# Moving value, inverse and weight transfers between the steps of a delta-rule scan

## The chip, the cores and the metric

The kernel runs on one core of a Trainium2 chip. The metric is the device time of one execution in microseconds (us).

## The reference

Attention with a delta-rule state over 32 (batch, head) pairs, 768 tokens and head size 48, and then two feed-forward layers over 3072 tokens, 384 features and 2048 hidden units. All is fp32.

```python
for t in range(S):                       # k_n: normalized keys
    y[:, :, t] = einsum('bhd,bhde->bhe', q[:, :, t], state)
    v_old = einsum('bhde,bhd->bhe', state, k_n[:, :, t])
    state = state + beta_t * einsum('bhd,bhe->bhde', k_n[:, :, t], v_t - v_old)
x = y as tokens x features
h = x @ w_in;  g = (a0 + a1*h + a2*h^2 + a3*h^3) / (1 + |b0|*|h| + |b1|*h^2 + 1e-6);  x = g @ w_out
h = x @ w2_in; r = max(h, 0);  result = (r * r) @ w2_out
```

## The kernel before

**The scan.** Tokens are cut into 48 chunks ("groups") of 64 tokens, 12 for each of 4 batches; a group holds 4 head pairs. Four groups are a quad (12 quads, 384 KB of keys, 384 KB of values, 768 KB of turned keys and queries each), eight are a round (6 rounds). Inside a chunk the recurrence becomes a triangular system. Its 32 x 32 diagonal blocks are inverted in place, a round at a time: round 0 on DVE ahead of the loop, rounds 1 to 5 on POOL (`invert`, L393 to L418, with L393 the first operation of a round). The rest is matmul work on PE in a loop of 50 steps, `for n in range(LAST_MM)`, which each engine runs in its own order with semaphores between them. In step n PE starts z of group n (L505), does y and the state of group n-2 (L549, L552), the cross product (L515), m and q of group n-1 (L535), the turned state (L563), the end of z (L521), and the key products of a group some 20 ahead (L484). ACT in the same step takes the products of a former step (L664), z_first (L672), the new state (L686, L687), the cross product (L678), y (L695) and the state (L709); at its end, in some steps, it spreads keys (L643, L645), squares and roots them (L623, L630). The cross product of a step on PE waits for z_first of the same step on ACT. In steps 2 to 7 the keys of half a quad are spread at the end of the step: in step 6 those of quad 7.

**The transfers.** All loads, and the stores of blocks and inverses, are issued from SP, in program order, with their waits in the same order; the stores of y go from ACT. For each step SP runs, in this order: `load_cross` and `load_q` (L308, L292), `load_kq` (L248), `store_n` (L266, L270), `store_inverse(r)` (L287), `load_blocks(r)` (L282), `load_inverse(h)` (L319), `load_k` (L236), `load_v` (L242), weights. `store_inverse(r)` waits for POOL's round r and stands in step `INV_OUT[r]`, that is 6, 13, 20, 27 and 34 for r = 1 to 5. `load_blocks(r)` brings round r to POOL, for r = 2 in step 6 and for r = 5 in step 27, each after the stores (`store_n`) of its quads. `load_kq(7)` stands in step 6, `store_n(11)` in step 26, values of quad 11 in step 34, `load_cross(11)` and `load_inverse(11)` in step 41. The rounds lie in three slots of 1024 columns in `shared[0]`.

**The feed-forward.** A layer is 96 units, 16 blocks of 128 hidden units for each of 6 tiles of 512 tokens. Weights, x and g are split in a high and a low part, and a unit has 9 matmuls up (L1123 to L1125) and 9 down (L1137 to L1139). Raw weights come in a ring of 4 slots of 768 columns in the same `shared[0]`; ACT splits off the high part (L1160), DVE the low one (L1247), into `weights`, which lies where quads 4 to 7, keys and queries were. In the first layer unit n goes through ACT (squares, L1171 to L1177), POOL (denominator, L1341, L1348), ACT (a guess at its reciprocal by Ln and Exp, L1184, L1188), DVE (head, L1270), POOL (L1355), DVE (L1275, L1282), and `up(n)` needs unit n-5 done (`g_lo_ready`). Nine weights (`PRE`) are split in steps 40 to 48 of the scan, the others in the first tile, one each unit. Up-projections of units 0 to 2 lie inside steps 46 to 48.

```python
if n == FF_LOADS:                        # 37
    ff.load_ab(sp)
    ff.load_weights(sp, 0)
    ff.load_x(sp, 0)
    for i in range(1, ff.W_SLOTS):
        ff.load_weights(sp, i)
if 0 <= n - FF_LOADS - 2 < ff.PRE:       # steps 39 to 47
    ff.load_weights(sp, n - FF_LOADS - 2 + ff.W_SLOTS)
```

From the fifth weight on `load_weights` waits on SP until DVE has split the former tenant of the slot.

Of the kernel before, what the change touches and what calls it, by code (L numbers as in the profile page):

```python
# [32 lines left out]
def build_attention(nc, dims, memory, banks, kq_in, k_in, v_in, beta_in, blocks_dram, inverse_dram, cross_dram, ff, x_out):  # L33
# [16 lines left out]
    RING = 32  # L50
# [2 lines left out]
    TWICE = (2, 8)  # L53
    LEAD = UPFRONT + TWICE[1] - TWICE[0]
    LAST_MM = GROUPS + 2
    FF_LOADS, FF_SPLIT, FF_X = GROUPS - 11, GROUPS - 8, (41, 43, 45)
    STORES = 16 * (SUB + 2)
    LOADS = 16 * (SUB + 3)
    INV_OPS = 2 * BL - 2
# [34 lines left out]
    with ExitStack() as ctx:  # L94
# [137 lines left out]
        def _(sp):  # L232
# [6 lines left out]
            def load_v(h):  # L239
                if h >= RING // 4:  # L240
                    sp.wait_ge(ys_done, 4 * h + 4 - RING)
                sp.dma_start(ring(h)[:, :, :, 0:D].rearrange("r g p d -> r (g p) d"),  # L242
                             v_in[:, QP * h:QP * h + QP, :]).then_inc(v_loaded[h % (RING // 4)], 16)
# [101 lines left out]
            load_blocks(1)  # L345
            load_k(6)
            load_k(7)
            load_v(2)
            for n in range(LAST_MM):
                for h in range(2, QUADS):  # L350
                    if n == 4 * h - 3:
                        load_cross(h)
                for h in range(6, QUADS):
                    if n == (2 * h - 8 if h < 9 else 4 * h - 26):
                        load_kq(h)
                for h in range(4, QUADS):
                    if n == step_of_quad(h):
                        store_n(h)
                for r in range(1, ROUNDS):
                    if n == INV_OUT[r]:  # L360
                        store_inverse(r)
                for r in range(2, ROUNDS):
                    if n == step_of_quad(2 * r + 1) + 1:
                        load_blocks(r)
                for h in range(2, QUADS):
                    if n == max(4 * h - 3, INV_OUT[h // 2]):
                        load_inverse(h)
                for h in range(8, QUADS):
                    if n == 4 * h - 26:
                        load_k(h)  # L370
                for h in range(3, QUADS):
                    if n == 4 * h - 10:
                        load_v(h)
                if n == FF_LOADS:
                    ff.load_ab(sp)
                    ff.load_weights(sp, 0)
                    ff.load_x(sp, 0)
                    for i in range(1, ff.W_SLOTS):
                        ff.load_weights(sp, i)
                if 0 <= n - FF_LOADS - 2 < ff.PRE:  # L380
                    ff.load_weights(sp, n - FF_LOADS - 2 + ff.W_SLOTS)
            ff.sync(sp)

        @block.gpsimd
# [233 lines left out]
        def _(act):  # L618
# [116 lines left out]
            for n in range(LAST_MM):  # L735
                if n > 0 and end_group(n - 1) is not None:
                    take_n(end_group(n - 1))
                if n < GROUPS:
                    take_z_first(n)
                if n in FF_X:  # L740
                    ff.split_x_hi(act, FF_X.index(n), 0)
                spread = (n + 1 + LEAD) // 2 if n > TWICE[1] and n % 2 == 1 and end_group(n + 1) is not None else None
                if spread is not None:
                    spread_keys(spread, (0,))
# [22 lines left out]
                        roots(norm_chunk(h))  # L767
                if n == 4 * QUADS - 24:
                    act.preload_act_table_set("natural_log_exp_and_others")
                if 0 <= n - FF_SPLIT < ff.PRE:  # L770
                    ff.split_weights_hi(act, n - FF_SPLIT)
                if n == GROUPS - 1:
                    ff.take_h(act, 0)
                if n == GROUPS:
# [5 lines left out]
        def _(dve):  # L780
# [158 lines left out]
            for n in range(LAST_MM):  # L939
# [20 lines left out]
                for h in range(2, QUADS):  # L960
                    if n == (1 if h == 2 else 4 * h - 5):
                        scale_v(h)
                if n == FF_SPLIT:
                    ff.coef_bounds(dve)
                if 0 <= n - FF_SPLIT < ff.PRE:
                    ff.split_weights_lo(dve, n - FF_SPLIT)
                if n in FF_X:
                    ff.split_x_lo(dve, FF_X.index(n), 0)
            ff.vector(dve, ys_done, GROUPS)


def build_feed_forward(nc, ctx, rows, moe_in, moe_out, coef_dram, memory, banks, x_first, x_second, out):
# [9 lines left out]

    LAG_RECIP, LAG_HEAD, LAG_LOW, LAG_DOWN = 1, 2, 3, 5
    H_BANKS, DEEP, TRIPLE, SHORT = 5, 4, 3, 2
    W_SLOTS, W_AHEAD, PRE = 4, 3, 9
    EARLY = {UNITS - 7: 0, UNITS - 5: 1, UNITS - 3: 2}

    def sem(name):
# [62 lines left out]
        return ps_h[n % H_BANKS]  # L1051

    def load_ab(sp):
        sp.dma_start(ab, coef_dram).then_inc(ab_loaded, 16)

    def load_weights(sp, i):
        m, f, slot = i // FT, i % FT, i % W_SLOTS
        if i >= W_SLOTS:  # L1060
            sp.wait_ge(w_lo_ready, i - W_SLOTS + 1)
        sp.dma_start(w_raw[:, slot, 0:D_MODEL].rearrange("p (k n) -> p k n", k=KT),
                     w_in_dram[m][:, :, f * P:(f + 1) * P]).then_inc(w_loaded[slot], 16)
        sp.dma_start(w_raw[:, slot, D_MODEL:2 * D_MODEL], w_out_dram[m][:, f, :]).then_inc(w_loaded[slot], 16)
# [88 lines left out]

    def split_weights_hi(act, i):
        f = i % FT
        act.wait_ge(w_loaded[i % W_SLOTS], 32 * (i // W_SLOTS) + 32)
        if i >= FT:
            act.wait_ge(h_ready, UNITS - FT + f + 1)
            act.wait_ge(down_done, UNITS - FT + f + 1)
        act.activation(weights[:, f, 0:2 * D_MODEL], w_raw[:, i % W_SLOTS], ACT.Copy).then_inc(w_hi_ready, 1)  # L1160

    def split_x_hi(act, k, tile):
        act.wait_ge(x_loaded, 16 * (tile + 1))
# [80 lines left out]
    def split_weights_lo(dve, i):  # L1244
        f = i % FT
        dve.wait_ge(w_hi_ready, i + 1)
        dve.tensor_tensor(weights[:, f, 2 * D_MODEL:4 * D_MODEL], w_raw[:, i % W_SLOTS],  # L1247
                          weights[:, f, 0:2 * D_MODEL].bitcast(F32), ALU.subtract).then_inc(w_lo_ready, 1)

    def split_x_lo(dve, k, tile):  # L1250
# [203 lines left out]
```

## Time and profile before

| | |
|---|---|
| median of 3 runs | 1114.39 us (1114.38 to 1116.54) |
| the profiled execution | 1114.34 us |
| its span, first to last instruction | 1112.6 us |
| PE busy | 1094.1 us (98%) |
| DVE, ACT, POOL busy | 678.0, 650.8, 509.2 us |
| mean granted TensorE clock | 0.994 |
| key products and scan loop | to about 327 us |
| the twelve feed-forward tiles | from there to the end |

Busy times count an engine from the start of an instruction to its modelled end; matmuls overlap, so their durations add up to more than the time. The granted clock is in parts of 2.4 GHz: 1.00 is the full and 0.50 the lower level.

### The profile page before, as it was taken

To read this page: it belongs to the slowest core of one execution; us is meant where nothing else is said; L and a number is where in the kernel's file an instruction comes from. 1 tells how busy PE (TensorE), PEld (TensorE's weight loads), DVE (VectorE), ACT (ScalarE), POOL (GpSimd) and SP (SyncE) were. 2 spreads that over 40 slices of the span, in tenths; PEclk is the share of its full clock that TensorE was granted. 3 is DMA by queue.
4 is the path that set the end of the run, shared out by engine and by line. 5 is a ranking of instruction groups with operands and counts; after the bars stand their busy time and mean duration, and the time that the engine had idled before them with its cause. 6 is when DMAs were issued, how large, how long until landed. Compare 5 with 4: busy or idle time off the path is not lost.

```text
span 1112.6 us, 18161 instructions
## 1 busy us (share of the span) xinstructions
PE 1094.1 (98%) x6372; PEld 944.5 (85%) x6372; DVE 678.0 (61%) x1088; ACT 650.8 (58%) x1275; POOL 509.2 (46%) x626
## 2 busy tenths in 40 slices
PE   8899999999999999999999999999999999999998
PEld 6699999999987788888888888888888888888887
DVE  6987564434559989787888879854333333434332
ACT  5566666544669777787877778653333323333322
POOL 5087888783039977887777878500000000000000
PEclk9799999999999999999999999999999999999999
DMA  8948887555531110100101002140100101010000
GB/s 193 204 84 182 165 180 151 117 94 149 135 107 57 44 57 1 32 27 1 57 1 57 1 22 93 43 128 1 57 1 9 49 1 57 0 57 1 1 29 29
DMA packets 173658, 74.41 MB, mean 67 GB/s; under 512 B 136000, under 2 KB 161728, under 8 KB 172608
## 3 DMA queue, kind: packets, MB, share of 16 engines
q1 hardware_dynamic: 163968, 68.54, 25.6%
q10 hardware_dynamic: 9600, 4.72, 1.7%
q8 instruction: 51, 0.84, 0.3%
q14 instruction: 39, 0.32, 0.1%
HBM read 52.27 MB, written 20.71 MB: 66 GB/s over the span
## 4 chain that ended last, share of the span: by engine, by line
PE 89%; DVE 6%; issue 2%; DMA 1%; POOL 1%; SPq 1%; ACT 0%; POOLq 0%; DVEq 0%; ACTq 0%
PE ps L1137 11%; PE ps L1139 11%; PE ps L1138 11%; PE ps L1123 11%; PE ps L1125 11%; PE ps L1124 11%; PE ps L505 3%; PE ps L484 3%; PE ps L549 3%; PE ps L535 3%; PE ps L552 3%; PE ps L515 3%; PE ps L521 2%; PE ps L467 1%; PE ps L563 1%
## 5 line engine op out<-in xcount | busy, mean ns | idle before, releaser
L1123 PE MATMUL ps<-x_split,weights 128*128 128x512 f32 x576 | 225.0, 391 | 3.8 <-DVE g_lo L1282 2.9
L1137 PE MATMUL ps<-g_hi,weights 128*128 128x512 f32 x576 | 224.1, 389 | 0.1
L1124 PE MATMUL ps<-x_split,weights 128*128 128x512 f32 x576 | 224.1, 389 | 0.0
L1125 PE MATMUL ps<-x_split,weights 128*128 128x512 f32 x576 | 224.1, 389 | 0.0
L1138 PE MATMUL ps<-g_lo,weights 128*128 128x512 f32 x576 | 224.1, 389 | 0.0
L1139 PE MATMUL ps<-g_hi,weights 128*128 128x512 f32 x576 | 224.1, 389 | 0.0
L1292 DVE TENSOR_TENSOR common<-common 128x512 f32<-128x512 f32 x96 | 66.4, 691 | 135.0 <-ACT common L1196 133.4
L1202 ACT ACTIVATE g_hi<-common 128x512 fp32r<-128x512 f32 x96 | 60.8, 633 | 141.8 <-PE ps L1139 137.3
L1123 PEld LDWEIGHTS ps<-x_split,weights 128*128 128x128 f32 x576 | 108.1, 188 | 27.9 <-DVE g_lo L1282 4.6
L1341 POOL TENSOR_SCALAR common<-common,b_abs 128x512 f32<-128x512 f32 x96 | 75.8, 789 | 116.1 <-ACT common L1171 116.1
L1355 POOL TENSOR_TENSOR common<-common,g_hi 128x512 f32<-128x512 f32 x96 | 124.4, 1296 | 9.5 <-DVE g_hi L1270 9.5
L1348 POOL TENSOR_TENSOR common<-common 128x512 f32<-128x512 f32 x96 | 124.5, 1297 | 8.0
L1137 PEld LDWEIGHTS ps<-g_hi,weights 128*128 128x128 f32 x576 | 108.1, 188 | 22.9 <-issue 0.4
L1125 PEld LDWEIGHTS ps<-x_split,weights 128*128 128x128 f32 x576 | 108.1, 188 | 22.5
L1138 PEld LDWEIGHTS ps<-g_lo,weights 128*128 128x128 f32 x576 | 108.1, 188 | 22.5
L1139 PEld LDWEIGHTS ps<-g_hi,weights 128*128 128x128 f32 x576 | 108.1, 188 | 22.4
L1124 PEld LDWEIGHTS ps<-x_split,weights 128*128 128x128 f32 x576 | 108.1, 188 | 22.2
L1196 ACT ACTIVATE common<-ps 128x512 f32<-128x512 f32 x96 | 57.4, 598 | 103.8 <-PE ps L1125 103.5
L1299 DVE TENSOR_TENSOR g_lo<-common,g_hi 128x512 fp32r<-128x512 f32 x96 | 66.3, 691 | 61.5 <-PE ps L1139 61.5
L1171 ACT ACTIVATE common<-ps 128x512 f32<-128x512 f32 x96 | 57.3, 597 | 72.6 <-PE ps L1125 71.9
L1258 DVE TENSOR_TENSOR common<-common,ps 128x512 f32<-128x512 f32 x96 | 65.8, 685 | 52.5 <-ACT common L1177 51.7
L408 POOL TENSOR_TENSOR shared<-shared,scan_x 128x30 f32<-128x30 f32 (+9 forms) x150 | 84.1, 560 | 11.7
(121 smaller groups left out, 1917.4 us busy)
## 6 DMA issues: line engine op xcount, KB each, us to landing
scan_late<-kq_in SPq DMA_DIRECT2D x10, 768.0 KB, 5.4
scan_late<-kq_in SPq DMA_DIRECT2D x16, 384.0 KB, 4.7
shared<-w_in SPq DMA_DIRECT2D x32, 192.0 KB, 2.5
shared<-w_out SPq DMA_DIRECT2D x32, 192.0 KB, 2.6
x_first<-y_t ACTq DMA_DIRECT2D x24, 192.0 KB, 2.9
shared<-x_first SPq DMA_DIRECT2D x6, 768.0 KB, 5.8
x_second<-shared SPq DMA_DIRECT2D x6, 768.0 KB, 4.2
shared<-x_second SPq DMA_DIRECT2D x6, 768.0 KB, 5.9
```

The source lines that it names most:

```text
L408: step = pool.tensor_tensor(rest, rest, part, ALU.add)
L1123: pe.matmul(bank(n), lo, x_hi[:, slot, k, :], start=(k == 0), stop=False)
L1124: pe.matmul(bank(n), hi, x_lo[:, slot, k, :], start=False, stop=False)
L1125: mm = pe.matmul(bank(n), hi, x_hi[:, slot, k, :], start=False, stop=(k == KT - 1))
L1137: pe.matmul(ps_y[m], lo, g_hi[:, d, :], start=(f == 0), stop=False)
L1138: pe.matmul(ps_y[m], hi, g_lo[:, s, :], start=False, stop=False)
L1139: mm = pe.matmul(ps_y[m], hi, g_hi[:, d, :], start=False, stop=(f == FT - 1))
L1292: dve.tensor_tensor(q[:, n % DEEP, :], r, r, ALU.mult).then_inc(act_ready, 1)
L1299: dve.tensor_tensor(g_lo[:, n % TRIPLE, :], q[:, d, :], g_hi[:, d, :].bitcast(F32), ALU.subtract).then_inc(g_lo_ready, 1)
L1341: pool.tensor_scalar(den_part[:, s, :], h_sq[:, s, :], b_abs[:, 1:2], ONE_EPS, ALU.mult, ALU.add).then_inc(den_part_ready, 1)
L1348: pool.tensor_tensor(q[:, n % DEEP, :], den_part[:, s, :], b0_h[:, s, :], ALU.add).then_inc(q_ready, 1)
L1355: pool.tensor_tensor(prod[:, n % SHORT, :], q[:, n % DEEP, :], g_hi[:, n % DEEP, :].bitcast(F32), ALU.mult).then_inc(prod_ready, 1)
```

## The change

SP asks for the values of quads 3 to 7 directly behind those of quad 2, ahead of its loop, where they stood in steps 2, 6, 10, 14 and 18. `store_inverse(r)` is the first thing in its step. The small coefficients and weight 0 are asked for in step 31, weight 1 in 32, x in 33, weights 2 and 3 in 35 and 36, 4 and 5 in 37, 6 and 7 in 39, and 8 to 13 in 42 to 47. Weights 0 to 9 are split in steps 33, 34, 36, 37 and 41 to 46, the three parts of x in steps 38, 39 and 40. Weights 2 and 3 come into the slots of 0 and 1, so that the other two slots, where round 5 of the inverses lies, are first written by weights 4 and 5; `raw_slot`, `raw_former` and `raw_loads` say which slot, whose split frees it, and how many loads it has had. `PRE` is 10: one weight less is split in the first tile.

```diff
@@ -53,7 +53,11 @@
     TWICE = (2, 8)
     LEAD = UPFRONT + TWICE[1] - TWICE[0]
     LAST_MM = GROUPS + 2
-    FF_LOADS, FF_SPLIT, FF_X = GROUPS - 11, GROUPS - 8, (41, 43, 45)
+
+    W_LOADS = {31: (0,), 32: (1,), 35: (2,), 36: (3,), 37: (4, 5), 39: (6, 7), 42: (8,), 43: (9,), 44: (10,), 45: (11,),
+               46: (12,), 47: (13,)}
+    W_SPLITS = {33: 0, 34: 1, 36: 2, 37: 3, 41: 4, 42: 5, 43: 6, 44: 7, 45: 8, 46: 9}
+    X_LOAD, X_SPLITS = 33, (38, 39, 40)
     STORES = 16 * (SUB + 2)
     LOADS = 16 * (SUB + 3)
     INV_OPS = 2 * BL - 2
@@ -345,8 +349,12 @@
             load_blocks(1)
             load_k(6)
             load_k(7)
-            load_v(2)
+            for h in range(2, RING // 4):
+                load_v(h)
             for n in range(LAST_MM):
+                for r in range(1, ROUNDS):
+                    if n == INV_OUT[r]:
+                        store_inverse(r)
                 for h in range(2, QUADS):
                     if n == 4 * h - 3:
                         load_cross(h)
@@ -356,9 +364,6 @@
                 for h in range(4, QUADS):
                     if n == step_of_quad(h):
                         store_n(h)
-                for r in range(1, ROUNDS):
-                    if n == INV_OUT[r]:
-                        store_inverse(r)
                 for r in range(2, ROUNDS):
                     if n == step_of_quad(2 * r + 1) + 1:
                         load_blocks(r)
@@ -368,17 +373,15 @@
                 for h in range(8, QUADS):
                     if n == 4 * h - 26:
                         load_k(h)
-                for h in range(3, QUADS):
+                for h in range(RING // 4, QUADS):
                     if n == 4 * h - 10:
                         load_v(h)
-                if n == FF_LOADS:
+                if n == min(W_LOADS):
                     ff.load_ab(sp)
-                    ff.load_weights(sp, 0)
+                for i in W_LOADS.get(n, ()):
+                    ff.load_weights(sp, i)
+                if n == X_LOAD:
                     ff.load_x(sp, 0)
-                    for i in range(1, ff.W_SLOTS):
-                        ff.load_weights(sp, i)
-                if 0 <= n - FF_LOADS - 2 < ff.PRE:
-                    ff.load_weights(sp, n - FF_LOADS - 2 + ff.W_SLOTS)
             ff.sync(sp)
 
         @block.gpsimd
@@ -737,8 +740,8 @@
                     take_n(end_group(n - 1))
                 if n < GROUPS:
                     take_z_first(n)
-                if n in FF_X:
-                    ff.split_x_hi(act, FF_X.index(n), 0)
+                if n in X_SPLITS:
+                    ff.split_x_hi(act, X_SPLITS.index(n), 0)
                 spread = (n + 1 + LEAD) // 2 if n > TWICE[1] and n % 2 == 1 and end_group(n + 1) is not None else None
                 if spread is not None:
                     spread_keys(spread, (0,))
@@ -767,8 +770,8 @@
                         roots(norm_chunk(h))
                 if n == 4 * QUADS - 24:
                     act.preload_act_table_set("natural_log_exp_and_others")
-                if 0 <= n - FF_SPLIT < ff.PRE:
-                    ff.split_weights_hi(act, n - FF_SPLIT)
+                if n in W_SPLITS:
+                    ff.split_weights_hi(act, W_SPLITS[n])
                 if n == GROUPS - 1:
                     ff.take_h(act, 0)
                 if n == GROUPS:
@@ -960,12 +963,12 @@
                 for h in range(2, QUADS):
                     if n == (1 if h == 2 else 4 * h - 5):
                         scale_v(h)
-                if n == FF_SPLIT:
+                if n == min(W_SPLITS):
                     ff.coef_bounds(dve)
-                if 0 <= n - FF_SPLIT < ff.PRE:
-                    ff.split_weights_lo(dve, n - FF_SPLIT)
-                if n in FF_X:
-                    ff.split_x_lo(dve, FF_X.index(n), 0)
+                if n in W_SPLITS:
+                    ff.split_weights_lo(dve, W_SPLITS[n])
+                if n in X_SPLITS:
+                    ff.split_x_lo(dve, X_SPLITS.index(n), 0)
             ff.vector(dve, ys_done, GROUPS)
 
@@ -982,7 +985,7 @@
 
     LAG_RECIP, LAG_HEAD, LAG_LOW, LAG_DOWN = 1, 2, 3, 5
     H_BANKS, DEEP, TRIPLE, SHORT = 5, 4, 3, 2
-    W_SLOTS, W_AHEAD, PRE = 4, 3, 9
+    W_SLOTS, W_AHEAD, PRE = 4, 3, 10
     EARLY = {UNITS - 7: 0, UNITS - 5: 1, UNITS - 3: 2}
 
     def sem(name):
@@ -1051,14 +1054,26 @@
         return ps_h[n % H_BANKS]
 
+    def raw_slot(i):
+        return i if i < 2 else (i + 2) % W_SLOTS
+
+    def raw_former(i):
+
+        return {2: 0, 3: 1}.get(i, i - W_SLOTS if i >= 6 else None)
+
+    def raw_loads(i):
+
+        return 1 if i < 2 else (i + 2) // W_SLOTS + (raw_slot(i) < 2)
+
+
 
     def load_ab(sp):
         sp.dma_start(ab, coef_dram).then_inc(ab_loaded, 16)
 
     def load_weights(sp, i):
-        m, f, slot = i // FT, i % FT, i % W_SLOTS
-        if i >= W_SLOTS:
-            sp.wait_ge(w_lo_ready, i - W_SLOTS + 1)
+        m, f, slot = i // FT, i % FT, raw_slot(i)
+        if raw_former(i) is not None:
+            sp.wait_ge(w_lo_ready, raw_former(i) + 1)
         sp.dma_start(w_raw[:, slot, 0:D_MODEL].rearrange("p (k n) -> p k n", k=KT),
                      w_in_dram[m][:, :, f * P:(f + 1) * P]).then_inc(w_loaded[slot], 16)
         sp.dma_start(w_raw[:, slot, D_MODEL:2 * D_MODEL], w_out_dram[m][:, f, :]).then_inc(w_loaded[slot], 16)
@@ -1153,11 +1168,11 @@
 
     def split_weights_hi(act, i):
         f = i % FT
-        act.wait_ge(w_loaded[i % W_SLOTS], 32 * (i // W_SLOTS) + 32)
+        act.wait_ge(w_loaded[raw_slot(i)], 32 * raw_loads(i))
         if i >= FT:
             act.wait_ge(h_ready, UNITS - FT + f + 1)
             act.wait_ge(down_done, UNITS - FT + f + 1)
-        act.activation(weights[:, f, 0:2 * D_MODEL], w_raw[:, i % W_SLOTS], ACT.Copy).then_inc(w_hi_ready, 1)
+        act.activation(weights[:, f, 0:2 * D_MODEL], w_raw[:, raw_slot(i)], ACT.Copy).then_inc(w_hi_ready, 1)
 
     def split_x_hi(act, k, tile):
         act.wait_ge(x_loaded, 16 * (tile + 1))
@@ -1244,7 +1259,7 @@
     def split_weights_lo(dve, i):
         f = i % FT
         dve.wait_ge(w_hi_ready, i + 1)
-        dve.tensor_tensor(weights[:, f, 2 * D_MODEL:4 * D_MODEL], w_raw[:, i % W_SLOTS],
+        dve.tensor_tensor(weights[:, f, 2 * D_MODEL:4 * D_MODEL], w_raw[:, raw_slot(i)],
                           weights[:, f, 0:2 * D_MODEL].bitcast(F32), ALU.subtract).then_inc(w_lo_ready, 1)
 
     def split_x_lo(dve, k, tile):
```

## Rows read from the trace of the kernel before

**Rows 1.** Busy time by stretch: us, PE, PEld, DVE, ACT, POOL, clock, DMA share, GB/s
```profile
60.00:70.00 10.00, 8.67 (x86) 8.54 (x86) 8.00 (x19) 5.46 (x14) 8.75 (x16) 1.00 0.01 3
...
110.00:120.00 10.00, 10.00 (x102) 9.77 (x101) 6.59 (x15) 6.91 (x21) 8.82 (x16) 1.00 1.14 211
```

**Rows 2.** SP queue, loop steps 4 to 6: start, us, engine, line, operation
```profile
74.10 0.34 SPq L248 DMA_DIRECT2D scan_late<-kq_in  x1
...
91.57 0.48 SPq L248 DMA_DIRECT2D scan_late<-kq_in  x1
...
95.00 0.34 SPq L287 DMA_DIRECT2D inverse_blocks<-shared  x1
95.52 0.34 SPq L282 DMA_DIRECT2D shared<-blocks  x1
```

**Rows 3.** Busy time of a stretch full of loads, columns as in group 1
```profile
97.00:99.00 2.00, 2.00 (x22) 2.00 (x22) 0.94 (x5) 2.00 (x8) 0.00 (x0) 1.00 0.86 295
```

**Rows 4.** ACT timeline, end of step 6; in brackets idle before, and releaser
```profile
96.80 0.72 ACT L643 ACTIVATE scan_late<-scan_late,scan_common 96x512 f32<-96x512 f32 x1 [0.97 <-DMA scan_late<-kq_in]
```

**Rows 5.** PE timeline, step 7
```profile
99.47 0.92 PE L515 MATMUL ps<-scan_common,scan_late 128*96 128x96 f32 x8
```

**Rows 6.** POOL timeline, the first operation of four rounds
```profile
53.88 2.36 POOL L393 TENSOR_TENSOR shared<-shared,scan_common 128x1024 f32<-128x1024 f32 x1 [34.89 <-DMA shared<-blocks]
...
100.28 2.36 POOL L393 TENSOR_TENSOR shared<-shared,scan_common 128x1024 f32<-128x1024 f32 x1 [5.31 <-DMA shared<-blocks]
...
139.84 2.35 POOL L393 TENSOR_TENSOR shared<-shared,scan_common 128x1024 f32<-128x1024 f32 x1
...
222.75 2.36 POOL L393 TENSOR_TENSOR shared<-shared,scan_common 128x1024 f32<-128x1024 f32 x1 [5.75 <-DMA shared<-blocks]
```

**Rows 7.** SP queue, loop step 34
```profile
261.61 0.34 SPq L287 DMA_DIRECT2D inverse_blocks<-shared  x1
262.00 0.43 SPq L242 DMA_DIRECT2D scan_x<-v_in  x1
```

**Rows 8.** ACT timeline, last operation of step 36 and the first weight split
```profile
261.46 0.49 ACT L709 ACTIVATE scan_common<-ps 96x384 f32<-96x384 f32 x1 [0.35 <-PE ps L563]
...
280.43 0.83 ACT L1160 ACTIVATE weights<-shared 128x768 fp32r<-128x768 f32 x1
```

**Rows 9.** PE timeline, cross product of step 37, starts of steps 42 to 44
```profile
264.38 0.84 PE L515 MATMUL ps<-scan_common,scan_late 128*96 128x96 f32 x8
...
285.43 1.06 PE L505 MATMUL ps<-scan_common 128*128 128x96 f32 x8
...
290.33 1.06 PE L505 MATMUL ps<-scan_common 128*128 128x96 f32 x8
...
296.15 1.13 PE L505 MATMUL ps<-scan_x,scan_common 128*128 128x96 f32 x8 [0.76 <-DMA scan_common<-inverse_blocks]
```

**Rows 10.** DVE, ACT and PE timelines, start of the feed-forward
```profile
324.24 0.96 DVE L1247 TENSOR_TENSOR weights<-shared,weights 128x768 fp32r<-128x768 f32 x1 [0.97 <-ACT weights L1160]
...
330.93 0.64 ACT L1184 ACTIVATE common<-common 128x512 f32<-128x512 f32 x1 [0.98 <-POOL common L1348]
...
338.29 0.50 PE L1123 MATMUL ps<-x_split,weights 128*128 128x512 f32 x1 [2.39 <-DVE g_lo L1282]
```

**Rows 11.** PE timeline, first matmul of two up-projections in the first tile
```profile
354.74 0.39 PE L1123 MATMUL ps<-x_split,weights 128*128 128x512 f32 x1
...
368.24 0.50 PE L1123 MATMUL ps<-x_split,weights 128*128 128x512 f32 x1 [0.25 <-DVE g_lo L1282]
```

**Rows 12.** PE timeline and stretches with the granted clock, before and after gaps
```profile
15.65 7.31 PE L484 MATMUL ps<-scan_late 96*128 96x128 f32 x64
...
25.87 5.47 PE L484 MATMUL ps<-scan_late 96*128 96x128 f32 x32 [2.91 <-ACT scan_late L645]
...
28.00:29.00 1.00, 1.00 (x7) 1.00 (x6) 0.89 (x4) 0.00 (x0) 0.00 (x0) 0.50 1.39 112
...
338.00:340.00 2.00, 1.71 (x7) 1.43 (x8) 1.98 (x4) 2.00 (x5) 2.00 (x3) 1.00 0.04 8
```

## The prediction

> **What bounds the kernel now.** I read the page first, then PE busy by stretches, then the PE, ACT, POOL and SP timelines of the places where PE is not full. In the scan a 10 us stretch has PE busy for all 10.00 [rows 1], and from step 9 to the first up-projection I find one PE stall only, at step 44. So an edit inside the scan gives time back only at a PE gap, and it costs time as soon as PE has to wait. The gaps that the change can touch are: 0.76 us at step 44, ended by the DMA that brings inverses [rows 9]; 2.39 us before unit 6 of the feed-forward, ended by a DVE g_lo [rows 10]; and the units around 360 us, whose starts are more than a PE-bound unit apart [rows 11]. SP is one queue in program order: a wait at its head holds back everything behind it. That is where the new order must be followed.
>
> **Early values.** Quads 4 to 7 leave their places in steps 6, 10, 14 and 18 and go behind quad 3, which SP already issued before the first wait of the loop. DMA is idle from 60 to 70 us (share 0.01) and SP's next load, of keys and queries of quad 6, goes out at 74.10 [rows 1, 2]. One such transfer has 384 KB; at the 295 GB/s that a load stretch moves [rows 3] four need 5.3 us, at half that rate 10.7 us: done by about 66 to 71 us. Cost nothing; without that gap it would be up to 10 us on quad 6. They gain nothing either: no PE gap stands where they stood.
>
> **Stores first.** INV_OUT is unchanged, so only the order inside a step changes. It matters at step 6. Before, SP issued keys and queries of quad 7 at 91.57, then waited for POOL, stored round 1 at 95.00 and loaded the blocks of round 2 at 95.52 [rows 2]. Now the store's wait is ahead of that load: it goes out at about 95.39, 3.8 us later, and the blocks at about 96.0, 0.5 us later. ACT has no room for this: it already sat 0.97 us until that load landed, at 96.80 [rows 4], after a flight of 5.2 us, and PE's next L515 started late behind it [rows 5]. Store, quad 7 and blocks are 512, 768 and 512 KB, 1.31 MB up to the end of quad 7 and 1.83 MB in all. At 295 GB/s [rows 3] that is 4.4 and 6.2 us of data. Of quad 7's old flight of 5.2 us 2.7 were data at that rate, so at most 2.5 lie around it; I take 1.8. Then quad 7 lands near 95.0 + 1.8 + 4.4 = 101.2 (4.4 late) and the blocks near 103.0 (POOL took up round 2 at 100.28 [rows 6], so 2.8 late). Bounds: quad 7 3.8 (same flight) to 5.1; blocks 0.5 (only the issue) to 5.2 (a whole flight behind quad 7). ACT is in order: behind the spread of keys stand the roots of quad 7 and the copies of step 7, so PE stops before L515 of step 7 for about 4.2 us. From there PE is 4.2 late. POOL runs its rounds back to back, so it stays 2.8 late; its one later wait, for the blocks of round 5 (restart at 222.75 [rows 6]), is behind a store of quad 11 that now is 4.2 late, about 3.0 in all. At step 13 the cross blocks and queries of quad 4 wait for the store too, three steps ahead of their use: nothing.
>
> **Weights from step 31 on.** Weights 0 and 1 and x are asked for in slots whose rounds were stored long ago. Weight 2 is asked for at step 35, behind the store of round 5 at step 34. SP came past that store only at 261.61 [rows 7], when POOL was done. ACT began its take_state of step 36 at 261.46 [rows 8], ended it near 261.9 and would turn to the split of weight 2 there. With POOL 3.0 late the store goes out at 264.6; then the values of quad 11, then both halves of weight 2 (the values were issued 0.39 us behind the store [rows 7]). The three make 1.31 MB, again 4.4 + 1.8: weight 2 lands 6.2 us after the end of the inversion (bounds: 4.0, an issue at 1.4 and the 2.6 of a transfer that overlaps all others; 8.0, the same data at the 211 GB/s of a mixed stretch [rows 1]), so at 270.8. Then split 0.74 (from its start to the next op's) and z_first 0.49 on ACT: PE's L515 of step 37 can start at about 272.1. It started at 264.38 [rows 9]: 7.7 late, of which 4.2 are the old delay and 3.5 a second stall. Queued behind the wait on ACT are z_first, the state and the y of step 37; PE waits for them. The other splits lie as those of steps 40 to 46 did, at 0.83 us on an ACT with idle time in each step [rows 8]: nothing, as long as their weights are there, and 3, 4 to 9 are asked for a step or more ahead.
>
> **What comes back.** The inverses of quad 11 were behind two weight waits; at step 41 none is there now. Steps 42 and 43 take 4.90 and 5.82 us [rows 9]: 0.9 back. Steps 47 and 48 lose their splits on ACT (0.74 each) and DVE. DVE's last split ran at 324.24, ahead of all its work for unit 0; from it the chain goes over head 0, POOL's product 0 and q 1 to ACT's Ln of unit 1 at 330.93 (0.98 idle for POOL), and, links later, to PE at 338.29 [rows 10]. With the splits gone head 0 is bounded by ACT's guess, 2.0 earlier; ACT is bounded by y of the last chunk and gains 1.35; prod 1 and so unit 6 about 1.4 (bounds 0.7, one split, and 2.4, the whole gap). Ten instead of nine weights split early takes one DVE split (0.96 [rows 10]) and one ACT split out of the first tile. Three units ran 368.24 - 354.74 = 13.50 [rows 11]; the four before ran 354.74 - 338.29 = 16.45, 4.11 each, so 3 x 4.11 = 12.33: 1.2 lost to DVE. I take all of it as back, since DVE also starts the tile 1.4 earlier; bound below 0.9.
>
> **Sum.** +7.7 - 0.9 - 1.4 - 1.2 = +4.2 on the span of 1112.6: 1116.8. The profiled execution took 1114.34, 1.74 more than its span, and lies 0.05 from the median of the runs, so 1118.5.
>
> **Clock.** The granted clock fell to 0.50, the lower of its two levels, at 28 to 29 us, after PE had been idle 2.91 us, and 32 matmuls took 5.47 us; after the 2.39 us gap at 338 it stayed at 1.00 [rows 12]. My two gaps (4.2 and 3.5) are longer than both. At the full level the 64 matmuls before took 7.31 [rows 12], so 32 take 3.6 and a fall costs 1.9. I count none in the sum: these gaps lie in dense work, as the one at 338 did, and not in the thin start. The Trainium skill, "TensorE: Matmul & The Clock Gate", section "Why this matters for your kernels", asks that PE not idle between bursts of matmuls because the clock then goes back to 1.2 GHz. By it each of the two gaps would cost a stretch at the lower level; the trace agrees at 28 us and not at 338.
>
> **The rivals.**
> 1. The clock falls after one or both gaps. For it: both are longer than the one that was followed by a fall, and the first is in matmuls of the same shape. A fall at step 7 is not absorbed, since it makes the stores of quad 11 and so round 5 later. 4.2 + 1.9 = +6.1, or +8.0: 1120.4 or 1122.3.
> 2. Only one wait shows. If quad 7 and the blocks are served together at full rate POOL is just 0.5 late, and if weight 2 lands 4.0 after the inversion it is there at 266.1, when an ACT that is 3.8 late arrives at 265.7. Then the delay stays 3.8 and 3.8 - 3.5 = +0.3: 1114.6; anything between gives up to +2. Against it: 768 and 512 KB in one queue.
> 3. Faster: POOL's rounds come out shorter. Round 1 took from 53.88 to the store at 95.00, 41.1 us, round 2 from 100.28 to 139.84, 39.6 [rows 2, 6], for the same instructions; the difference is single ops stretched beside DVE work. With quad 7 on time the whole depends on POOL being done by 91.6 in round 1 and before 258 in round 5 (3.5 us sooner, each from there on). Then only the returns are left: -3.5, 1110.8. It decides (by 2.2 us) from a delay at step 37 below 1.3. Against it: nothing in the change touches POOL's work or when it starts.
> 4. Nothing changes, since all moved transfers were hidden: excluded at step 6 by ACT's 0.97 us wait.
>
> **How the numbers follow.** Two late loads without a clock fall 0.41; with a fall 0.24; only one wait shows 0.24; faster 0.11. This kernel tells 0.2%, 2.2 us, from no change: up to 1112.2 is faster, from 1116.6 slower. Case 2 is the same. The sum's own bounds: lowest +0.3; highest, POOL 5.2 late, weight 2 8.0 after it and 2.5 back: 7.7 + 2.2 + 1.8 - 2.5 = +9.2. The range leaves out the faster case and double falls: 1114.4 to 1122.0. The main case alone: 1116.8 to 1120.0.
>
> **What would show it.** Right: SP's load of quad 7 issued right behind the store near 95.4; ACT idle before L643 some 5 us instead of 0.97, a PE gap near 4 us before L515 of step 7; POOL's second L393 near 103; ACT idle before a weights split with the DMA of w_out as releaser near 271, and a PE gap of 3 to 4 us; no idle before step 44; the gap before unit 6 near 1.3. Wrong: POOL restarting at 100.8, no ACT wait at the split of weight 2, or a clock below 1.00 behind either gap.

## The result and the profile after

The changed kernel took 1124.62 us (median of 4, 1124.45 to 1124.9), the one before, beside it, 1115.47 us (median of 4, 1114.38 to 1117.54). The ratio is 1.0087 (95% interval 1.0075 to 1.0099): 9.2 us slower. The forecast was 1118.5 us, with a range of 1114.4 to 1122.0, so the time lies 2.6 us above the range. The profiled execution took 1124.9 us, its span grew from 1112.6 to 1123.2.

The page of the changed kernel, its span, PE's busy time and PE's granted clock in 40 slices:

```profile
span 1123.2 us, 18161 instructions
...
PE 1095.7 (98%) x6372; PEld 947.3 (84%) x6372; DVE 677.8 (60%) x1088; ACT 650.5 (58%) x1275; POOL 508.4 (45%) x626
...
PEclk9898999998999999999999999999999999999999
```

PE's busy time is nearly what it was (1094.1 before), so the added time is PE idle, in two places, plus slower matmuls behind them: the clock's fourth and tenth slices show 8s where there were 9s.

**The first gap.** The SP queue in step 6, columns start and duration in us, engine, line, operation (line numbers are 3 to 4 higher than before, in the feed-forward 15):

```profile
93.81 0.34 SPq L291 DMA_DIRECT2D inverse_blocks<-shared  x1
94.20 0.43 SPq L252 DMA_DIRECT2D scan_late<-kq_in  x1
94.80 0.65 SPq L286 DMA_DIRECT2D shared<-blocks  x1
96.85 1.91 SPq L323 DMA_DIRECT2D scan_common<-inverse_blocks  x4
```

The store of round 1 now stands ahead of quad 7's keys and queries, as forecast: that load goes out 0.39 us behind the store where it was 3.4 us ahead of it [rows 2]. ACT's spread of these keys in the same step, PE's cross product of step 7 and the key products behind it, POOL's round 2:

```profile
101.57 0.72 ACT L646 ACTIVATE scan_late<-scan_late,scan_common 96x512 f32<-96x512 f32 x1 [6.90 <-DMA scan_late<-kq_in]
```

```profile
104.23 1.59 PE L518 MATMUL ps<-scan_common,scan_late 128*96 128x96 f32 x8 [6.08 <-ACT scan_common L675]
106.46 2.05 PE L487 MATMUL ps<-scan_late 96*128 96x128 f32 x8 [0.63 <-DVE scan_late L857]
```

```profile
103.59 2.35 POOL L396 TENSOR_TENSOR shared<-shared,scan_common 128x1024 f32<-128x1024 f32 x1 [9.81 <-DMA shared<-blocks]
```

ACT sits 6.90 us where it sat 0.97 [rows 4], and PE is idle for 6.08 us ahead of L518. Between L518 and its old start [rows 5] lie 4.8 us, and this execution was 1.2 us earlier until then, so the gap cost 5.9 us. POOL takes up round 2 at 103.59 against 100.28 [rows 6]: 3.3 us later, 4.5 with the 1.2.

**The second gap.** SP in step 34 and 35, ACT's split of weight 2 in step 36, and three cross products on PE, the second of which is that of step 37:

```profile
268.76 0.34 SPq L291 DMA_DIRECT2D inverse_blocks<-shared  x1
269.14 0.43 SPq L246 DMA_DIRECT2D scan_x<-v_in  x1
269.62 2.09 SPq L1077 DMA_DIRECT2D shared<-w_in  x1
271.76 0.49 SPq L1079 DMA_DIRECT2D shared<-w_out  x1
```

```profile
274.87 0.84 ACT L1175 ACTIVATE weights<-shared 128x768 fp32r<-128x768 f32 x1 [5.76 <-DMA shared<-w_out]
```

```profile
266.64 0.84 PE L518 MATMUL ps<-scan_common,scan_late 128*96 128x96 f32 x8
...
276.14 1.60 PE L518 MATMUL ps<-scan_common,scan_late 128*96 128x96 f32 x8 [4.44 <-ACT scan_common L675]
...
282.33 0.89 PE L518 MATMUL ps<-scan_common,scan_late 128*96 128x96 f32 x8
```

The order is that of the forecast: store of round 5, values of quad 11, weight 2 in two halves. SP needed 2.09 us to issue the first half. ACT stood idle for 5.76 us until the second half had landed, and PE for 4.44 us. POOL's round 5 had begun at 228.61, where it began at 222.75 [rows 6]:

```profile
228.61 2.36 POOL L396 TENSOR_TENSOR shared<-shared,scan_common 128x1024 f32<-128x1024 f32 x1 [8.15 <-DMA shared<-blocks]
```

Round 5 also took longer. From its start to its store it was 40.15 us, before 38.86. Two of its operations stand beside the DVE splits of weights 0 and 1, which the change moved to steps 33 and 34, and took 1.27 and 1.10 us instead of 0.61 and 0.51. The first of the two, before and after, and the DVE split next to it:

```profile
249.71 0.61 POOL L408 TENSOR_TENSOR shared<-shared,scan_x 128x220 f32<-128x220 f32 x1
...
255.73 1.27 POOL L411 TENSOR_TENSOR shared<-shared,scan_x 128x220 f32<-128x220 f32 x1
...
255.59 0.95 DVE L1262 TENSOR_TENSOR weights<-shared,weights 128x768 fp32r<-128x768 f32 x1
```

**The clock.** Stretches of the changed kernel; columns: stretch, its length, busy time and count of PE, PEld, DVE, ACT, POOL, granted clock, DMA share, GB/s:

```profile
102.00:104.00 2.00, 0.00 (x0) 0.00 (x0) 0.85 (x4) 2.00 (x8) 0.41 (x1) 0.50 0.98 97
106.00:108.00 2.00, 1.54 (x7) 1.57 (x8) 1.27 (x6) 0.62 (x2) 1.59 (x6) 0.50 0.00 0
110.00:112.00 2.00, 2.00 (x20) 2.00 (x19) 1.32 (x2) 1.38 (x3) 1.76 (x4) 0.90 0.67 123
112.00:114.00 2.00, 2.00 (x22) 2.00 (x21) 2.00 (x3) 1.57 (x6) 1.76 (x4) 1.00 1.27 230
275.00:276.00 1.00, 0.00 (x0) 0.00 (x0) 0.26 (x1) 1.00 (x2) 0.00 (x0) 0.50 1.17 251
276.00:278.00 2.00, 1.86 (x11) 1.86 (x12) 0.70 (x1) 0.32 (x2) 0.00 (x0) 0.50 1.24 208
282.00:284.00 2.00, 2.00 (x24) 2.00 (x23) 0.37 (x1) 2.00 (x6) 0.00 (x0) 1.00 1.10 332
```

The clock is at 0.50 already at the end of both gaps, while PE is idle, and back at 1.00 by 112 and by 282 us. Each of the two L518 rows behind a gap lasts 1.6 us, about twice the usual 0.84.

**What came back.** No stall stands before step 44. The gap before unit 6 of the feed-forward is 0.97 us instead of 2.39 [rows 10]:

```profile
349.63 0.50 PE L1138 MATMUL ps<-x_split,weights 128*128 128x512 f32 x1 [0.97 <-DVE g_lo L1297]
```

The account of the two profiled spans, from starts of the same instruction (after minus before): opening -1.2; step 7 +5.9, the clock and a DVE collision behind it +2.7, step 9 -0.3; gap at step 37 +4.6 and the clock behind it +2.4; step 44 -1.0; from the last cross product to unit 6 -1.8 (11.61 us to the next up-projection and 9.44 from there, where it was 11.99 and 10.85); the tiles -0.7. The sum is +10.6, within rounding.

### The profile page after: what moved, and what is told of

Read it like the earlier page. It is cut to its first block, busy times and chain, and to the rows that moved or that the text cites. A ratio compares the mean times of both kernels' runs of the same rounds, so it can differ in the third digit from the quotient of the medians.

```text
span 1123.2 us, 18161 instructions
## 1 busy us (share of the span) xinstructions
PE 1095.7 (98%) x6372; PEld 947.3 (84%) x6372; DVE 677.8 (60%) x1088; ACT 650.5 (58%) x1275; POOL 508.4 (45%) x626
## 4 chain that ended last, share of the span: by engine, by line
PE 84%; POOL 7%; DMA 3%; DVE 2%; issue 2%; SPq 2%; ACT 1%; ACTq 0%; POOLq 0%; DVEq 0%
PE ps L1152 11%; PE ps L1154 11%; PE ps L1153 11%; PE ps L1138 11%; PE ps L1140 11%; PE ps L1139 11%; POOL shared L411 3%; POOL scan_x L406 3%; PE ps L487 2%; PE ps L538 2%; PE ps L508 2%; PE ps L552 2%; PE ps L524 2%; PE ps L555 2%; PE ps L518 2%
```

## The experiments

Each run has the kernel before on the same chip beside it; differences are to that one's median unless another is named. Those times of before were 1114.8, 1114.77, 1115.0 and 1115.12 us. The changed kernel's 1124.62 us belongs to the 1115.47 above and was not taken again beside the later runs, so a difference to it can be off by a few tenths.

**The parts alone.** The early values alone:

```diff
-            load_v(2)
+            for h in range(2, RING // 4):
+                load_v(h)
...
-                for h in range(3, QUADS):
+                for h in range(RING // 4, QUADS):
                     if n == 4 * h - 10:
                         load_v(h)
```

> The kernel before with the early values alone. Theory (two late loads and two falls of the clock, none of it from the values): the four transfers land in the DMA idle time near 60 to 68 us, so the time is that of before, within 0.5 us. Rival (the early values crowd the next loads, quad 6's keys and queries or the blocks, and bring part of the loss): 1 to 4 us slower, with an ACT wait on quad 6 near 78 us.

Measured: 1113.29 us, ratio 0.9989 (0.998 to 0.9998), 1.5 us faster. It is not a loss, and it is more gain than either theory gave; the last runs below take it up.

The stores first, alone:

```diff
             for n in range(LAST_MM):
+                for r in range(1, ROUNDS):
+                    if n == INV_OUT[r]:
+                        store_inverse(r)
...
-                for r in range(1, ROUNDS):
-                    if n == INV_OUT[r]:
-                        store_inverse(r)
```

> The kernel before with the stores of inverses first in their step and nothing else. Theory: the first PE gap of about 6 us before the cross product of step 7 and a fall of the clock behind it come back in full, +5.9 and +2.4, so 8.3 us slower than before; the inverses of quad 11 at step 44 still wait (0.9). Rival A (the gap needs the other edits, for instance the DMA load of the early values): no more than the 1 us that step 7 lost before. Rival B (no clock cost, only the gap): +5.9.

Measured: 1122.35 us, ratio 1.0065 (1.0053 to 1.0078), 7.6 us slower. PE's timeline at step 7:

```profile
104.80 1.60 PE L515 MATMUL ps<-scan_common,scan_late 128*96 128x96 f32 x8 [6.42 <-ACT scan_common L672]
```

The gap of the changed kernel is there with nothing else changed, so it needs neither the early values nor the weights. Rival A falls. The loss is also above the gap alone, which speaks for a cost of the clock but is within the spread of a few tenths to a microsecond that such sums have. From the cross product of step 7 to that of step 8 PE took 10.2 us, as in the changed kernel, and 7.5 before.

This trace also bears on the row that the forecast's choice on the clock rests on, the gap before unit 6 with no fall behind it [rows 12]. Here the same gap is as long, and the clock did fall:

```profile
346.41 0.80 PE L1123 MATMUL ps<-x_split,weights 128*128 128x512 f32 x1 [2.37 <-DVE g_lo L1282]
...
347.00:349.00 2.00, 2.00 (x6) 1.62 (x5) 1.99 (x5) 1.97 (x4) 1.92 (x3) 0.50 0.03 8
```

The new places of weights and x alone (stores and values as before):

```diff
-                if n == FF_LOADS:
+                if n == min(W_LOADS):
                     ff.load_ab(sp)
-                    ff.load_weights(sp, 0)
+                for i in W_LOADS.get(n, ()):
+                    ff.load_weights(sp, i)
+                if n == X_LOAD:
                     ff.load_x(sp, 0)
...
```

> The kernel before with the new places of weights and x alone, stores and values where they were. Theory: POOL ends round 5 near 261.6 as before, weight 2 lands 6.1 us later near 267.8, so ACT waits about 6 us at its split in step 36, PE some 4.7 us before the cross product of step 37, the clock falls behind it (+2.4), and 1.0 at step 44, 1.8 at the start of the feed-forward and 0.7 in the first tile come back: 3.6 us slower than before. Rival A (weight 2 is late only because step 7 made POOL and the stores late): no wait, 3.5 us faster. Rival B (the clock does not fall after a gap of this size): +1.2.

Measured: 1116.74 us, ratio 1.0018 (1.0009 to 1.0027), 1.9 us slower. ACT's split of weight 2 and PE's cross product of step 37 in this kernel:

```profile
267.08 0.84 ACT L1174 ACTIVATE weights<-shared 128x768 fp32r<-128x768 f32 x1 [5.01 <-DMA shared<-w_out]
```

```profile
268.36 1.59 PE L517 MATMUL ps<-scan_common,scan_late 128*96 128x96 f32 x8 [3.69 <-ACT scan_common L674]
```

Weight 2 is late with step 7 undisturbed, which rules out rival A. It landed 6.1 us after its round's store at 260.98, the same distance as in the changed kernel (268.76 to 274.87). Round 5 took 40.0 us, and 39.8 to 40.8 in all nine kernels with the new places, against 38.6 to 39.0 in the five without: the DVE splits beside it are the weights' doing. The gap was 3.69 where I had expected 4.7: before it this execution lost 0.9 us in step 9, and what PE loses ahead of a gap that POOL ends is not lost twice. The clock fell here too, but was low for less long: from the cross product of step 14 to that of step 47 this kernel took 177.95 us, and kernels without a stall there (below) 172.57; of the 5.4 us between, 1.7 are not the gap. So the loss is 1.9 and not 3.6.

The changed kernel with the stores back at the end of their step:

```diff
-                for r in range(1, ROUNDS):
-                    if n == INV_OUT[r]:
-                        store_inverse(r)
                 for h in range(2, QUADS):
...
+                for r in range(1, ROUNDS):
+                    if n == INV_OUT[r]:
+                        store_inverse(r)
                 for r in range(2, ROUNDS):
```

> The changed kernel with the stores of inverses back behind the other transfers of their step; early values and weights as changed. Theory: the same as with the weights alone, 3.6 us slower than before, and no gap at step 7 beyond that of before. Rival (early values bring a loss of their own beside the new weights): slower than weights alone by more than 0.5 us.

Measured: 1117.85 us, ratio 1.0028 (1.0017 to 1.004), 3.1 us slower, 1.1 more than the weights alone although the early values by themselves gain. The gap on PE explains the absent gain:

```profile
269.92 1.59 PE L518 MATMUL ps<-scan_common,scan_late 128*96 128x96 f32 x8 [5.47 <-ACT scan_common L675]
```

5.47 us where the weights alone have 3.69. POOL and the transfers behind its store set the moment at which this gap ends, so a PE that comes earlier waits longer. The gap ended 1.6 us later than with the weights alone (268.36), because POOL began round 5 at 222.61 instead of 220.94: its blocks took 5.2 us to land instead of 4.2, and the rest was there before. Why that flight differs no run shows.

**The clock.** Matmuls whose results nobody reads, into a bank that the next cross product overwrites, ahead of the cross products of steps 7 and 37 in the changed kernel:

```diff
+                if n in {7: 14, 37: 10}:
+                    for _ in range({7: 14, 37: 10}[n]):
+                        pe.matmul(banks[1][:, 0:PAIRS * D2], ident, neg_cross[:, :, :].rearrange("r p d -> r (p d)"),
+                                  start=True, stop=True)
                 if n < GROUPS:
                     cross_z(n)
```

> The changed kernel with matmuls on old data in the two gaps, 14 ahead of the cross product of step 7 and 10 ahead of that of step 37, 384 columns each, into a bank that the cross product overwrites; 4.9 and 3.5 us at 0.35 us each, both less than the gaps of 6.1 and 4.4. Their results are not used. Theory (each gap costs its own length and, behind it, a stretch at the lower clock, 2.4 us each): the granted clock stays at 1.00 behind both and the time falls by 4.8 us against the changed kernel, to about 1119.8. Rival (the clock falls in the records, but the scan is paced by something else and the slower part is latency): no change, or slower by the added work.

and the same with `{7: 14}`, the first gap alone:

> The changed kernel with the 14 matmuls in the first gap only. Theory: round 5's blocks wait for stores of quad 11 that PE paces, so 2.4 us taken out behind step 7 reach the second gap's end too: 2.4 us faster than the changed kernel. Rival (round 5 and weight 2 are paced by POOL alone): the second gap grows by the 2.4 us and the time stays.

Measured: 1124.29 and 1124.43 us, no gain over 1124.62. Both tell little, since I had sized the filler by a wrong row. The first row is the 14 filler matmuls, the second the cross product behind them:

```profile
98.56 9.21 PE L599 MATMUL ps<-scan_common 128*128 128x384 f32 x28
107.61 0.58 PE L518 MATMUL ps<-scan_common,scan_late 128*96 128x96 f32 x5
```

Each is two records and takes 0.65 us; 14 take 9.05 us and overrun the gap by about 3. The clock did stay at 1.00. So I ran them shorter, with `{7: 8, 37: 5}`:

> The two kernels with matmuls in the gaps had 0.65 us for each of them, not 0.35, since one fp32 matmul of 384 columns is two passes: 9.05 us in a gap of 6.1. They kept the clock at 1.00 and overran the gap by 3.0. Now 8 ahead of step 7's cross product (5.2 us) and 5 ahead of step 37's (3.25 us), both shorter than the gaps; their results are not used. Theory: no overrun and no fall of the clock, 4.8 us faster than the changed kernel, near 1119.8. Rival (the lower clock cost nothing, as the steps behind a gap are bound by latency): 1124.6 as before.

Measured: 1120.96 us, 3.7 us faster than the changed kernel (ratio to before 1.0053, 1.0041 to 1.0066). The filler of step 7, and stretches that answer to those at 0.50 above:

```profile
99.06 5.34 PE L599 MATMUL ps<-scan_common 128*128 128x384 f32 x16
```

```profile
102.00:104.00 2.00, 2.00 (x8) 1.11 (x6) 1.02 (x1) 2.00 (x8) 1.08 (x1) 1.00 1.39 165
106.00:108.00 2.00, 1.51 (x14) 1.54 (x15) 1.69 (x9) 0.00 (x0) 1.61 (x6) 1.00 0.00 0
276.00:278.00 2.00, 2.00 (x23) 2.00 (x22) 1.90 (x3) 1.56 (x3) 0.00 (x0) 1.00 1.47 150
```

The clock stays at 1.00, and the rival falls. (The trace shows two records for each filler; that they are passes, as I put it above, it does not say.) From the cross product of step 6 to that of step 8 PE took 20.2 us instead of 23.2, from step 14 to step 47 176.9 instead of 179.5: 2.9 and 2.6 us. The first of these also holds 1.1 us that are not the clock's, since quad 7 landed 6.6 us after the store instead of 7.7. From the cross product behind each gap to the next one, which leaves the gaps out, it is 8.3 instead of 10.2 us and 3.9 instead of 6.2: the falls cost 1.9 and 2.3 us. The medians give 3.7 for both (3.2 when each is taken against its own kernel before), less than the 4.8 expected; the opening of this execution was 0.8 us later than that of the changed kernel.

**Round 5's store out of the way.** Stores at the end of their step, early values and new weight places kept, and

```diff
-    INV_OUT = (None, 6, 13, 20, 27, 34)
+    INV_OUT = (None, 6, 13, 20, 27, 37)
```

> Early values and the new weight places, stores of inverses at the end of their step as before, and round 5's store in step 37 instead of 34, so that weights 2 and 3 and the values of quad 11 go out ahead of it. Theory: no gap at step 37, none at step 44; only the returns are left, 1.0 + 1.8 + 0.7 = 3.5 us faster than before, near 1111.3. Rival (the inverses of quad 10 now land too late, as their store goes out some 2 us later): a new PE wait of up to 2 us at step 40 by the DMA of the inverses, 1.5 us faster at most.

Measured: 1109.64 us, ratio 0.9953 (0.9941 to 0.9966): 5.1 us faster than before and 15 us under the changed kernel's 1124.62. That is more than the 3.5 expected, and not the rival's 1.5 or less. The forecast of it gave the early values nothing; they are taken up below. SP in steps 34 to 37 (values of quad 11, weight 2's two halves, store of round 5), and ACT's split of weight 2, which has no idle time in front of it:

```profile
247.29 0.48 SPq L246 DMA_DIRECT2D scan_x<-v_in  x1
247.81 3.55 SPq L1077 DMA_DIRECT2D shared<-w_in  x1
251.41 0.49 SPq L1079 DMA_DIRECT2D shared<-w_out  x1
...
262.71 0.34 SPq L291 DMA_DIRECT2D inverse_blocks<-shared  x1
```

```profile
260.12 0.83 ACT L1175 ACTIVATE weights<-shared 128x768 fp32r<-128x768 f32 x1
```

The first half of weight 2 goes out 15 us ahead of POOL's end instead of behind it, and the inverses of quad 10 are still in time: PE has no stall from step 8 to the first feed-forward units. The same line changed in the changed kernel, with its stores first:

> The changed kernel with nothing but round 5's store in step 37 instead of 34; stores stay first in their step. Theory: the first gap and its fall stay (+8.3), the second gap and its fall go, so it is the best version plus 8.3 us, 1118 (6.9 us faster than the changed kernel, which is 4.5 of gap and 2.4 of clock). Rival (the two losses are one, and the second appears elsewhere, at step 40 by the inverses of quad 10): 1121 or more.

Measured: 1118.27 us, ratio 1.0027 (1.0019 to 1.0036), 6.35 us faster than the changed kernel. From step 14 to step 47 the kernels with the late store took 172.57 us, the changed one 179.53: 6.96 us for gap and clock of step 37 together. The two losses are separate.

**Which store.** The kernel before, with the stores first for rounds 2 to 5 only:

```diff
+                for r in range(2, ROUNDS):
+                    if n == INV_OUT[r]:
+                        store_inverse(r)
...
-                    if n == INV_OUT[r]:
+                    if n == INV_OUT[r] and r == 1:
```

> The kernel before with the stores first in their step for rounds 2 to 5 but not for round 1. Theory (the whole cost of stores first is quad 7 behind the store of round 1 in step 6): the time of before, within 0.5 us. Rival (quad 4's cross blocks, which now wait for the store of round 2 in step 13, are late too): a PE wait at step 16 and 1 us or more slower.

Measured: 1114.88 us, ratio 1.0002 (0.9993 to 1.001): no change. The whole cost of that part is round 1's store in step 6. Its profile is of one of the two slowest of its 11 runs (1116.74). It has a stall that the one of before hardly had, on ACT in step 9, where the keys of quad 8 are spread; PE is idle for 2.45 us by it, and the clock falls to 0.50 behind:

```profile
115.08 0.72 ACT L646 ACTIVATE scan_late<-scan_late,scan_common 96x512 f32<-96x512 f32 x1 [3.53 <-DMA scan_late<-kq_in]
```

**What the early values give.** The best version without them:

> The best version without the early values: they stand in steps 2 to 18 again. Theory (the values are hidden either way): within 1 us of the version with them, near 1110. Rival (the early values give 1.5 us of their own, as their own run's median suggests): near 1111.2, and in the trace a longer step 7, 8 or 9 than with them.

Measured: 1111.61 us, ratio 0.9966 (0.9952 to 0.9979), 2.0 us slower than with them. The same stall on ACT, and SP from the values of quad 4 (L246) over the block stores (L270) to the keys of quad 8 (L252):

```profile
115.46 0.72 ACT L645 ACTIVATE scan_late<-scan_late,scan_common 96x512 f32<-96x512 f32 x1 [2.53 <-DMA scan_late<-kq_in]
```

```profile
101.70 1.47 SPq L246 DMA_DIRECT2D scan_late<-v_in  x1
103.31 5.16 SPq L270 DMA_DIRECT2D blocks<-shared  x4
...
109.62 0.48 SPq L252 DMA_DIRECT2D scan_late<-kq_in  x1
```

The four block stores take 5.16 us to issue behind the values of quad 4 (2.82 with them gone, in the version above), and the keys go out at 109.62. From the cross product of step 9 to that of step 10 PE took 6.08 (before), 6.72 (weights alone), 7.53 (this one) and 10.16 us (stores from round 2) in the four kernels that have quad 4's values in step 6 and no gap at step 7, and 5.80 in every one that asks for them early. Against 5.80 the four losses are 0.3 to 4.4 us, 1.8 on average; each is of one execution. Last, quads 3 and 4 alone ahead of the loop, on the kernel before:

> The kernel before with the values of quad 4 (and of quad 3, which went out at the same time anyway) ahead of the loop; quads 5 to 7 stay in steps 10, 14 and 18. Theory: the gain of the early values comes from step 6 alone. There quad 4's values stood ahead of the block stores of step 7 and the keys of quad 8 behind them, and ACT waited 1.1 to 3.5 us for those keys in step 9; now it waits 0.6 us at most, step 9 takes 5.80 us on PE, and the time is that of all early values, some 1.5 us below before. Rival (the gain is from quads 5 to 7 or is noise of the opening): the time of before and a step 9 of 6 us or more.

Measured: 1113.24 us, ratio 0.9981 (0.9972 to 0.999), 1.9 us faster, at least as much as all early values. Its step 9 took 5.80 us.

```profile
112.63 0.72 ACT L645 ACTIVATE scan_late<-scan_late,scan_common 96x512 f32<-96x512 f32 x1 [0.79 <-DMA scan_late<-kq_in]
```

So quad 4's values alone, moved from step 6, give the gain. ACT waits 0.79 us, which PE does not feel. The stall of step 9 differs between executions, so it may be part of the spread of the kernel before (1113.34 to 1117.98 over 22 runs); no run shows it.

## Why the prediction was wrong

**Early values.** The cover was as said: the four loads were issued from 56.5 to 63.2 us and nothing waited for them. "They gain nothing either: no PE gap stands where they stood" was wrong. I had read 0.3 us at step 9 as nothing and did not ask what stood behind quad 4's values in the queue. Behind them it is a stall of 0.3 to 4.4 us, by execution, and the part is worth 1.5 to 2.0 us.

**Stores first.** The mechanism is confirmed by the stores alone and by rounds 2 to 5 alone: quad 7's keys behind the store of round 1. Two sizes were off. From the store to the landing of quad 7 I took 6.2 us, 4.4 of data and 1.8 around it; it was 7.7 (93.81 to 101.55), and the loss at step 7 5.9 instead of 4.2. The six kernels with this order had 6.6 to 8.1 us, so 6.2 was low, and some of the miss is spread. The store had landed after 3.0 us, so that the 64 KB loads of inverses went out at 96.85, still inside quad 7's flight, where before they had come behind it; that they slowed it is argued, not shown. POOL restarted 4.5 us late on its own time instead of 2.8.

**Weights.** The chain through SP, the 6.2 us from the store to the landing (6.1) and the place of the gap were right. The gap was 4.6 instead of 3.5. Round 5 began 5.9 us later instead of 3.0, since it waits for stores that PE paces; but PE itself came to step 37 7.2 us later instead of 4.2, so this alone leaves the gap as forecast. What made it longer is that round 5 took 1.3 us more, beside the two DVE splits. I had put that at nothing, with "nothing in the change touches POOL's work" under rival 3: the moved splits do.

**Clock.** This is the step that failed: "I count none in the sum". I went by the gap of 2.39 us at 338 us, in dense work; but both new gaps were longer than the 2.91 us at 23 us that a fall had followed, and the first stood in matmuls of that same kind. That was the nearer row. The row at 338 us was no assurance even for its own length: the same gap has a fall behind it in the stores alone. The falls cost 1.9 and 2.3 us behind their gaps in the profiles, and 3.7 together in the medians. The price of 1.9 in the prediction was right; what failed was to leave it out. The time left the range by 2.6 us, and without the falls it would have lain in it. The two gaps were 1.7 and 1.1 us longer than forecast; had only these come out as forecast, the time would have been about 1121.8, just inside. So the clock is the largest of the misses and not the only one. Rival 1, with two falls, had the mechanism and 1122.3 for it, with a chance that also held the single fall. The Trainium skill, "TensorE: Matmul & The Clock Gate", section "Why this matters for your kernels", asks for no idle gaps above a certain length between bursts of matmuls; the changed kernel's trace agrees at both gaps. The 2.39 us at 338 us [rows 12] are shorter than the length that it names, so the prediction was wrong to hold them against it; the fall behind 2.37 us in the stores alone differs from it the other way.

**Returns.** 0.9, 1.4 and 1.2 were forecast, 1.0, 1.8 and 0.7 measured, 3.5 in all both times: the y of the last chunk also came 0.4 earlier, and DVE was not quite out of the way in the tile.

**Against the rivals.** Rival 2 (one wait) and 3 (POOL's rounds shorter) did not come about: POOL's rounds 2 to 4 took 38.7 to 39.1 us, before 38.1 to 39.6, and round 5 came out longer.

## What to carry to other kernels

In a queue that serves several consumers in order, a store that waits for a slow engine is placed behind everything that others need before that engine is done; here the places of two such stores make most of the difference between 9 us slower and 5 us faster. Read each transfer of a step for what stands behind it, even if no stall shows at its own place. A PE gap longer than one after which the clock has already fallen in the same trace is to be priced with the fall, and a gap without a fall in one execution is no proof that the next has none. Work moved to another engine's stretch can slow that engine: look what runs beside it there.

## What the runs showed of the hardware

- The granted clock fell to 0.50 while PE was still idle, in gaps of 6.08 and 4.44 us, and was back at 1.00 about 6 and 5 us after the work had resumed. Filler matmuls in the gaps kept it at 1.00.
- Behind 60 us of the span, a fall came in or just behind all seven PE gaps of 3.69 to 6.42 us in these traces, two of the six of 2.33 to 2.45 us (stores alone at 346 us, stores from round 2 at 116 us), and none shorter than 1.5 us.
- One fp32 matmul of 384 columns shows as two records and takes 0.65 us.
- Behind a load in pieces of 192 bytes (48 fp32 of each head) SP needed 2.1 us (3.6 in the version with the late store) to issue a 192 KB transfer that mostly takes 0.4 to 0.5, and 3.6 to 5.2 us for four 64 KB stores that take 2.8 to 3.4 without that load ahead.
- A 128 x 16 DVE operation, of a form that takes 0.17 us elsewhere, took 2.23 us when it started 0.16 us behind POOL's 2.35 us operation on 1024 columns, as a 128 x 64 one had taken 2.40 in the kernel before. In the other direction, POOL operations of 0.5 to 0.6 us took 1.1 to 1.3 beside a DVE split of 128 x 768.
